# Splitting an attention stage's loads over two queues, and its weight pieces into thirds

## The reference

```python
for t in range(S):
    kt, vt, rt = (k[:, :, t], v[:, :, t], r[:, :, t])
    cur = np.einsum('bhd,bhe->bhde', u[None] * kt, vt)
    y[:, :, t] = np.einsum('bhd,bhde->bhe', rt, state + cur)
    state = w[None, :, :, None] * state + np.einsum('bhd,bhe->bhde', kt, vt)
```

## Time and profile before

| | |
|---|---|
| median of 3 runs | 302.24 us (301.41 to 302.4) |
| the profiled execution | 301.77 us, its span 300.0 us |
| mean granted TensorE clock | 0.968 |
| busy: PE, VectorE, ScalarE, GpSimd | 277.9, 161.8, 72.0, 62.3 us |
| attention, first to last `xs` copy | 21.0 to 129.3 us |
| moved by DMA | 52.57 MB, mean 175 GB/s |

### The profile page before, as it was taken

How to read it: one execution, slowest core, us unless ns; L and a number is a source line. 1 busy time by engine, 2 the same in 40 slices (tenths; PEclk the granted TensorE clock), 3 DMA queues, 4 the chain that set the end, 5 groups by cost and what they waited for, 6 DMA issues and landing times.

```text
span 300.0 us, 11059 instructions
## 1 busy us (share of the span) xinstructions
PE 277.9 (93%) x4821; PEld 237.5 (79%) x4821; DVE 161.8 (54%) x293; ACT 72.0 (24%) x150; POOL 62.3 (21%) x67
## 2 busy tenths in 40 slices
PE   8688399999999999999999989999999999999992
PEld 8576288888888788864334968999999999999992
DVE  5956428787878888753340238643352433525312
ACT  1002013223322332241102316323222222222200
POOL 3725205544564475050000000000000000000000
PEclk9959859999999999999999999999999999999998
DMA  5966926999999999887894090002020020200203
GB/s 150 250 137 211 294 82 204 302 347 258 332 276 320 340 271 367 289 309 309 306 418 174 8 391 23 2 1 105 0 95 10 0 105 0 105 0 0 105 3 110
DMA packets 13957, 52.57 MB, mean 175 GB/s; under 512 B 2032, under 2 KB 5296, under 8 KB 12144
## 3 DMA queue, kind: packets, MB, share of 16 engines
q1 hardware_dynamic: 12928, 41.28, 44.0%
q10 hardware_dynamic: 1008, 11.01, 9.4%
HBM read 47.56 MB, written 4.72 MB: 174 GB/s over the span
## 4 chain that ended last, share of the span: by engine, by line
PE 83%; DVE 4%; issue 3%; DMA 2%; ACT 1%; SPq 1%; DVEq 0%
PE ps L1094 11%; PE ps L1093 11%; PE ps L1095 11%; PE ps L885 10%; PE ps L865 6%; PE ps L876 5%; PE ps L837 4%; PE ps L1078 4%; PE ps L965 4%; PE ps L988 4%; PE ps L844 3%; PE ps L855 3%; PE ps L890 3%; DMA wraw<-wb 2%; DVE rkb L574 2%
## 5 line engine op out<-in xcount | busy, mean ns | idle before, releaser
L1094 PE MATMUL ps<-w2l,hh 128*128 128x384 f32 x192 | 64.5, 336 | 0.0
L1093 PE MATMUL ps<-w2h,hh 128*128 128x384 f32 x192 | 64.4, 336 | 0.0
L1095 PE MATMUL ps<-w2h,hl 128*128 128x384 f32 x192 | 64.3, 335 | 0.0
L753 DVE SCALAR_TENSOR_TENSOR hl<-ps,hh 128x512 fp32r<-128x512 f32 x48 | 32.9, 690 | 57.3 <-ACT hh L513 57.2
L513 ACT ACTIVATE hh<-ps 128x512 fp32r<-128x512 f32 x48 | 28.5, 598 | 74.7 <-PE ps L1078 74.7
L403 POOL TENSOR_TENSOR rk<-ind 112x512 f32<-112x512 f32 x24 | 30.9, 1287 | 55.1 <-PE ps L844 45.2
L1094 PEld LDWEIGHTS ps<-w2l,hh 128*128 128x128 f32 x192 | 36.0, 188 | 1.7
L1093 PEld LDWEIGHTS ps<-w2h,hh 128*128 128x128 f32 x192 | 36.0, 188 | 0.6
L1095 PEld LDWEIGHTS ps<-w2h,hl 128*128 128x128 f32 x192 | 36.1, 188 | 0.0
L574 DVE TENSOR_TENSOR rkb<-ind,tab 112x1024 f32<-112x1024 f32 x24 | 33.4, 1392 | 0.2
L885 PE MATMUL ps<-ident,xs 112*128 112x112 f32 x200 | 30.5, 299 | 0.0
(11 more groups left out here) (159 smaller groups left out, 347.3 us busy)
## 6 DMA issues: line engine op xcount, KB each, us to landing
wearly<-wa ACTq DMA_DIRECT2D x7, 1536.0 KB, 8.8
intk<-tmaj SPq DMA_DIRECT2D x24, 384.0 KB, 6.9
ind<-dmaj SPq DMA_DIRECT2D x44, 192.0 KB, 7.3
wearly<-wa SPq DMA_DIRECT2D x4, 1536.0 KB, 10.5
out<-acc SPq DMA_DIRECT2D x5, 768.0 KB, 3.5
wlate<-wa SPq DMA_DIRECT2D x4, 768.0 KB, 5.1
wlate<-wa SPq DMA_DIRECT2D x2, 1536.0 KB, 8.7
wmid<-wa SPq DMA_DIRECT2D x1, 1536.0 KB, 6.5
```

Of the source, the lines that this page charges most:

```text
L753: v.scalar_tensor_tensor(out=hl[:, f % 4, :], in0=ps[:, f % 4, :], scalar=0.0, in1=hh[:, f % 4, :].bitcast(F32), op0=ALU.max, op1=ALU.subt ...
L1093: mm(o, a_h, w2h[:, f, :], start=(f == 0), stop=False)
L1094: mm(o, a_h, w2l[:, f, :], start=False, stop=False)
L1095: ins = mm(o, a_l, w2h[:, f, :], start=False, stop=(f == KF - 1))
```

## The change

The second half of each `ind` load moves from SyncE's queue to ScalarE's: for steps 0 to 3 at the head of ScalarE's program, for step n + 4 at the top of its step n, behind the same two waits. The seven early weight pieces are loaded as 21 thirds of 128 partitions x 4 KB, one after each `xs` copy of steps 1 to 21, and PE's wait counts 21 loads. SyncE keeps the first halves, `intk` and everything after.

```diff
--- before.py
+++ after.py
@@ -265,6 +265,10 @@
             if count > 0:
                 engine.wait_ge(s, count)
 
+        def step_of(t, n):
+            at_ = n // PAIRS + n % PAIRS * NC
+            return t[at_:at_ + 1]
+
         def one(t, i):
             return t[0:1, bass.ds(i, 1)]
 
@@ -278,14 +282,12 @@
         @block.sync
         def _(sp):
             def load_d(n):
-                src = dmaj[n // PAIRS + n % PAIRS * NC:n // PAIRS + n % PAIRS * NC + 1]
+
                 low = HB if n < 4 else D
-                sp.dma_start(ind[0:low, n % 4, :, :], src[:, 0:low, 0:2]).then_inc(ind_in[n % 4], 16)
-                sp.dma_start(ind[HB:R2, n % 4, :, :], src[:, D:2 * D, 0:2]).then_inc(ind_in[n % 4], 16)
+                sp.dma_start(ind[0:low, n % 4, :, :], step_of(dmaj, n)[:, 0:low, 0:2]).then_inc(ind_in[n % 4], 16)
 
             def load_t(n):
-                src = tmaj[n // PAIRS + n % PAIRS * NC:n // PAIRS + n % PAIRS * NC + 1]
-                sp.dma_start(intk[:, n % 4, :, :, :], src).then_inc(tok_in[n % 4], 16)
+                sp.dma_start(intk[:, n % 4, :, :, :], step_of(tmaj, n)).then_inc(tok_in[n % 4], 16)
 
             sp.dma_start(wusb[0:HB, :, :], wu[0:HB]).then_inc(wu_in, 16)
             sp.dma_start(wusb[HB:R2, :, :], wu[D:2 * D]).then_inc(wu_in, 16)
@@ -423,6 +425,17 @@
         @block.scalar
         def _(sc):
             a = nc.scalar
+
+            def load_d(n):
+                sc.dma_start(ind[HB:R2, n % 4, :, :], step_of(dmaj, n)[:, D:2 * D, 0:2]).then_inc(ind_in[n % 4], 16)
+
+            def load_third(i):
+                p, w = i // 3, PIECE // 3
+                cols = slice(i % 3 * w, (i % 3 + 1) * w)
+                sc.dma_start(piece[p][:, cols], wa[p, :, cols]).then_inc(wpre, 16)
+
+            for n in range(4):
+                load_d(n)
             for s, n in starts["act"].items():
                 sc.sem_inc(s, n)
             sc.wait_ge(wkT_done, 1)
@@ -444,6 +457,10 @@
                              ACT.Copy).then_inc(lts_ready, 1)
 
             for n in range(STEPS):
+                if n + 4 < STEPS:
+                    sc.wait_ge(pre_ready, n + 1)
+                    sc.wait_ge(rk_ready, n + 1)
+                    load_d(n + 4)
                 if n:
                     sc.wait_ge(t_done, n + 1)
                     tok_copy(n - 1)
@@ -454,8 +471,8 @@
                 a.activation(xs[0:R2, :, :].rearrange("p b (m t) -> p m b t", m=2),
                              ps[0:R2, YB:YB + 2, 0:B * HALF].rearrange("p m (b t) -> p m b t", b=B),
                              ACT.Copy).then_inc(xs_ready, 1)
-                if n % 3 == 1 and n // 3 < 7:
-                    sc.dma_start(piece[n // 3], wa[n // 3]).then_inc(wpre, 16)
+                if 1 <= n <= 21:
+                    load_third(n - 1)
 
             sc.wait_ge(lg_done, STEPS + 1)
             lts_copy(NC - 1)
@@ -999,7 +1016,7 @@
                 ins.then_inc(ct_done, 1)
 
             pe.wait_ge(sit_ready, 1)
-            pe.wait_ge(wpre, 7 * 16)
+            pe.wait_ge(wpre, 21 * 16)
             layer1(0)
             layer1(1)
             turn_h(0)
```

## The result

The changed kernel took 300.85 us in the median of 20 runs (297.15 to 305.0), the kernel before 302.69 in 20 runs beside them (300.59 to 305.96). The ratio of the two is 0.9897, with a 95% interval of 0.9869 to 0.9926: some 3.1 us faster, where 9.2 were forecast. The ratio leaves out executions more than 1.5% above the fastest of their kernel, which are 9 of the changed kernel's 20 and 1 of the other's; over all twenty the medians are 1.8 us apart and the means 1.9.

What follows compares the result with a forecast made beforehand. PE was taken as the bound after 47.8 us, DMA hard behind, with code stops and half clock earlier. Gains of 6.9 + 0.3 + 2.0 = 9.2 us from 302.24 gave 293.0 us, range 289.0 to 300.0.

Steps and rivals of the forecast that it cites:

- part 5: Step 3 of the attention loop: PE's code stop falls from 4.92 to 1.34 us, clock stays full, 6.9 us gained.
- the place: Steps 3 and 4 of the attention loop: PE's long stop plus the half clock behind it, put at 8.2 us.
- part 4: Kernel start: four high halves issued at once from ScalarE; taken as 0, ends 1.7 us gained or lost.
- the first stop: PE's stop at 24.87 us in the attention loop, 0.78 us long: should lose 0.3 us, ends 0 and 0.78.
- part 6: Attention loop from 47.79 to 128.72 us: 2.0 of 2.7 us lost to late loads regained, ends 0 and 2.7.
- My first rival: Step 3: the clock falls all the same after a stop of, say, 2.5 us; total 297.5 us, chance 0.16.
- Part 1: Attention loop loads: ind halves in two queues meet at 406 GB/s, so a step needs 3.2 us of DMA, not 4.19.
- Part 3: ScalarE in the loop: two DMA issues after each xs, 0.8 to 2.0 us, cost nothing.
- The halves serialize: Rival, loop loads: ind still costs 1.93 us a step, stop of 3 us and half clock; 300.3 us, chance 0.12.
- The stops have nothing to do with DMA: Rival, PE's stops in steps 1 to 3: only 2.0 to 2.7 us gained; total 299.9 us, chance 0.10.
- Small packets: Rival, loop loads: thirds go at 260 GB/s and the old stop stays; total 307.1 us, chance 0.07.
- if I read them rightly: Doubt whether PE's stops in steps 1 to 3 are waits for the next 16 KB of code; total otherwise 299.9 us.

Runs made afterwards that it cites:

- b1: Kernel of loads alone, nothing of the reference computed: first halves of ind 137 GB/s, both halves in one queue 212, in two queues 232.
- e1: Changed kernel, with ScalarE waiting for the table's own small load before its first four second halves: median 300.46 us, ratio 0.988 to the kernel before.
- e2: Kernel before with the 21 thirds alone after steps 1 to 21, both ind halves on SyncE: median 300.28 us, ratio 0.988 to the kernel before.
- g1 to g3: Changed kernel unaltered, three further single profiled executions: 300.49, 301.52 and 303.49 us.
- g4: Kernel before with thirds alone after steps 1 to 21, both ind halves on SyncE, one execution: 295.73 us.
- e4: Kernel before with its seven whole weight pieces issued after steps 4, 7, 10, 13, 16, 19, 21: median 299.31 us, ratio 0.9856 to the kernel before.
- e6: Kernel before with thirds alone, issued after steps 3 to 23, both ind halves on SyncE: median 297.9 us, ratio 0.988 to the kernel before.

## Why the prediction was wrong

The sign was right and the size was not: 9.2 us forecast, 3.1 measured, 300.85 outside 289 to 300. Two steps of the prediction failed: part 5 took for granted that a stop of 1.34 us leaves the clock at full, and took the price of the place from one execution; part 4 put the start at nothing. The means of the table, four executions before and five of the changed kernel, give the sum as it came out. The start lost 4.1 us. Steps 0 to 2 gave 1.8 of it back. Steps 2 to 4 gained 2.4, where part 5 had 7.2 with its 0.3 for the first stop. Steps 4 to 23 gained 3.3, where part 6 had 2.0. The rest of the kernel lost 0.2. Together that is 3.2 us gained. With four and five executions, whose steps 4 to 23 spread over 4.7 and 2.0 us, the terms behind the start are good to 1 or 2 us, not better.

- **Part 4, the start.** I took 0 with ends of 1.7 either way and named the mechanism of the loss, "the table's own small load held up behind the new ones". It measured 4.1 us at the first `xs`, and 2.3 are left at that of step 2. My bound was PE's 1.68 us of waiting, which bounds a gain and says nothing of a loss; the loss is how late the first link of VectorE's chain can come. VectorE's first copy was 2.9 us late (3.18 to 6.11). An estimate from the earlier trace rows would have come near that, a half of 197 KB at 204 GB/s taking 0.96 us and three of them 2.9; but no run shows how many stood ahead, and b1 has halves alone at 137 GB/s. And the table's load is not the whole mechanism: with it landed in time (e1) first `xs` still stood at 23.31, as step 0's own `ind` and `wgsb` were late.
- **Part 5, the stop.** This is the largest miss, 2.4 us in place of 7.2. The mechanism held: thirds alone shorten the stop (1.47 and 2.17), whole pieces alone keep it (5.18), no weights in the first pass nearly remove it (0.52), and the instruction packet shows why. The stop was somewhat longer than sized, 1.34 forecast, 1.62 to 2.72 seen, mean 2.0. What failed first is "I take it that 1.34 does too", of the clock. In three of five executions of the changed kernel half clock followed, and 2 to 4 took 2.6 to 3.3 us more, 1.7 in the mean of the five; it followed stops of 1.47 in e2 and 1.62 in e1 as well. My first rival had this and I gave it 0.16. What failed next is the base: the 6.9 us were counted against the one execution of the kernel before that had a stop of 4.92, and 2 to 4 took 16.6 us there but 14.5 in the mean of the four, 2.2 less. The gain is 4.1 where the clock stays and 1.2 in g1 to g3.
- **Part 6, late loads**, 2.0 forecast: 1.9 and 1.4 against the first profile, and 3.3 between the means (2.9 with g1 to g3 alone). The mechanism, `kt` late by `intk`, is seen above, and the size is about right; but the forecast's own base, 2.7 us lost in the first profile, was a low one, and the credit goes to the thirds: e2 and g4 have 79.12 and 79.29 without any half moved.
- **Part 1, the halves together at 406 GB/s**, is refuted: 232 in two queues, 212 in one. The DMA share stays at 1.03. It did not spoil the sum: thirds alone bring the loop as near to PE's 4.05 us a step as the whole change does. The moved halves are the part of the change that costs.
- **Part 3, ScalarE's time**, cost nothing, as said: in the first profile its second issue took up to 1.64 us and no `xs` was late by it.
- **The rivals.** "The halves serialize" (232 GB/s, and the DMA share at 1.03) and "the clock falls all the same" (three of five) are both true to a degree; I had them as alternatives to the forecast when each could take its piece of it. "The stops have nothing to do with DMA" is refuted by e4. "Small packets" is refuted too: they cost 4% in loads alone, 416 GB/s at 4 KB against 433 at 12 KB. The doubt whether the stops are code at all ("if I read them rightly") is settled by the packets.

What is not settled: why the kernels' executions part in the way that they do. The programs of the kernel before, e2, e4 and e6 are the same up to the end of step 1, and first `xs` stood at 21.02, 20.88, 21.36 and 18.52, that of step 1 at 26.27, 28.50, 29.53 and 29.70. And what decides whether the clock falls behind a stop of 1.5 to 2.7 us is open. The profiles of the two kernels come mostly from different chips, so that a difference between chips is not kept out of their comparison: with g1 to g3 alone the mean spans differ by 1.3 us (301.4 and 300.1), with all five by 3.2.

## What to carry to other kernels

A small load that starts the longest chain must be out, and landed, before the bulk; bulk moved to a second queue no longer waits for what stands in the first, and can delay it. Cut a large prefetch that runs beside latency-bound loads into pieces of a step's size, and keep it out of the first pass of a loop, when the code is still coming. And before costing a stall from one profile, look at a second one of the same kernel: the place that cost 8.2 us in the first profile cost 5.1 to 5.5 in the three others.

## What was unexpected of the hardware

- A load to 48 partitions, 4 KB each, ran at 137 and 159 GB/s where one to 128 partitions ran at 416 (the loads are 192 and 512 KB, and no run parts size from span); two of them, in different partitions and different queues, at 232.
- The second issue in a row on a queue was slow at times: 1.64 us on ScalarE and 1.68 on SyncE at 35.1 us, when the DMA share was 1.0 and PE waited for code, against 0.38 and 0.39 us later in the loop, where the share is 1.03.
- After stops of nearly the same length the granted clock stayed at full in some executions (1.62 and 1.65 us) and went to half in others (1.47 in e2, 1.62 in e1, 1.90, 2.17, 2.57 and 2.72). It stayed behind all three under 1 us (0.52, 0.79, 0.94) and fell behind all five over 3 us.
- A packet of 16 KB of instructions took 1.1 to 1.7 us to move, PE went on 1.2 to 1.7 us after its end, and it began some 4 us later with whole weight pieces in flight than with no weights.
